# Two tiles of each layer's first bucket that load before the last scatters, four slot buffers, scatters without a bounds check, and a front without its surplus group

## The reference

```python
w = softmax(weight)                                   # 8 heads x 7 taps
x1[s, h] = sum over k of w[h, k] * x[s + k - 6, h]    # causal convolution, 24 numbers a head

do = x1 @ w_skip > 0                                  # first mixture layer, only these tokens
e  = argmax(x1 @ gate1);  g = softmax(...)[e]
x2 = x1 + do * g * (relu(x1 @ w1[e]) @ w2[e])         # 8 experts, 192 -> 1024 -> 192

e  = argmax(x2 @ gate2);  g = softmax(...)[e]         # second mixture layer, every token
out = g * sigmoid(x2 @ out_gate2)[e] * (relu(x2 @ w1'[e]) @ w2'[e])
```

## Time and profile before

| | us |
|---|---|
| median of 3 runs (lowest, highest) | 1117.85 (1116.25, 1118.25) |
| the profiled execution | 1117.96 |
| its span, first to last instruction | 1116.2 |
| PE busy in the span | 1048.8 |
| POOL busy in the span | 381.1 |
| mean granted PE clock | 0.976 of full |

### The profile page before, as it was taken

One profiled execution on the slowest core, in us unless ns is written; L12 is line 12 of the kernel. 1 busy time (PEld: TensorE's weight loads), 2 busy tenths in 40 slices (PEclk: granted clock), 3 DMA queues, 4 the chain that ended last, 5 costly groups with the idle time before them and its releaser, 6 DMA issues.

```text
span 1116.2 us, 32024 instructions
## 1 busy us (share of the span) xinstructions
PE 1048.8 (94%) x8478; PEld 988.4 (89%) x8479; DVE 704.9 (63%) x2258; ACT 528.4 (47%) x1190; POOL 381.1 (34%) x420
## 2 busy tenths in 40 slices
PE   7887747999999999999699999999999999999997
PEld 6666636999999999999599999999999999999997
DVE  1556654887878888888655555565656555565554
ACT  3445532444545454544245454554545455455443
POOL 2677773232323333333222232222323223223212
PEclk9999977999999999999899999999999999999999
DMA  7855334443433344344253343433434343323222
GB/s 209 241 184 156 101 121 117 98 101 71 96 75 93 89 97 98 82 95 110 71 131 81 75 114 65 113 81 79 113 79 111 64 101 93 65 58 73 61 60 49
DMA packets 252866, 110.90 MB, mean 99 GB/s; under 512 B 170515, under 2 KB 247814, under 8 KB 252848
## 3 DMA queue, kind: packets, MB, share of 16 engines
q1 hardware_dynamic: 210344, 62.19, 26.7%
q0 software_dynamic: 14560, 27.96, 7.1%
q10 hardware_dynamic: 27944, 20.57, 6.8%
HBM read 79.48 MB, written 33.08 MB: 101 GB/s over the span
## 4 chain that ended last, share of the span: by engine, by line
PE 83%; issue 7%; POOL 5%; DVE 2%; ACT 1%; DMA 1%; ACTq 1%; POOLq 0%; SPq 0%; DVEq 0%
PE bank L1104 32%; PE bank L1119 26%; PE bank L1126 12%; PE bank L1095 5%; POOL buckets L440 5%; PE bank L1066 2%; PE bank L1065 1%; PE bank L1054 1%; PE bank L1055 1%; PE bank L963 1%; PE bank L982 1%; DMA buckets<-rows,slot_i 0%; PE bank L1026 0%; ACT rows L527 0%; PE bank L1027 0%
## 5 line engine op out<-in xcount | busy, mean ns | idle before, releaser
L1119 PE MATMUL bank<-w,hh 128*128 128x384 f32 x1488 | 444.4, 361 | 0.4 <-DVE hl L821 0.4
L1126 PE MATMUL bank<-w,hl 128*128 128x192 f32 x1488 | 363.9, 255 | 0.0
L821 DVE SCALAR_TENSOR_TENSOR hl<-bank,hh 128x512 fp32r<-128x512 f32 x372 | 252.8, 690 | 126.7 <-ACT hh L615 123.9
L615 ACT ACTIVATE hh<-bank 128x512 fp32r<-128x512 f32 x372 | 221.6, 599 | 161.0 <-PE bank L1104 147.4
L1126 PEld LDWEIGHTS bank<-w,hl 128*128 128x128 f32 x1488 | 282.9, 191 | 0.0
L1119 PEld LDWEIGHTS bank<-w,hh 128*128 128x128 f32 x1488 | 280.4, 188 | 1.5 <-DVE hl L821 0.6
L466 POOL DMA_INDIRECT out<-y_rows,out_i x120 | 117.3, 978 | 413.4 <-DVE out_i L899 382.1
L1104 PE MATMUL bank<-xAh,w1h 128*128 128x256 f32 x744 | 222.5, 299 | 0.0
L1104 PE MATMUL bank<-xAh,w1l 128*128 128x256 f32 x744 | 210.2, 283 | 0.0
L1104 PE MATMUL bank<-xB,w1h 128*128 128x256 f32 x744 | 208.8, 281 | 0.0
L1104 PE MATMUL bank<-xAl,w1h 128*128 128x256 f32 x744 | 208.4, 280 | 0.0
(11 more groups left out here) (157 smaller groups left out, 1367.2 us busy)
## 6 DMA issues: line engine op xcount, KB each, us to landing
xblocks<-buckets SPq DMA_DIRECT2D x570, 32.0 KB, 1.8
xkeep<-buckets ACTq DMA_DIRECT2D x93, 196.0 KB, 2.7
xwin<-x SPq DMA_DIRECT2D x17, 672.0 KB
raw<-w_all SPq DMA_DIRECT2D x56, 192.0 KB
raw<-w_all SPq DMA_DIRECT2D x56, 128.0 KB
raw<-w_all SPq DMA_DIRECT2D x112, 64.0 KB
out<-y_rows,out_i POOLq DMA_INDIRECT x120
buckets<-rows,slot_i POOLq DMA_INDIRECT x112
```

Of the source, the lines that this page charges most:

```text
L615: nc.scalar.activation(hh[:, 2 * c:2 * c + 2, :].rearrange("p c t -> p (c t)"), bank[c][:], ACT.Relu).then_inc(s["h_high"], 1)
L821: nc.vector.scalar_tensor_tensor(hl[:, 2 * c:2 * c + 2, :].rearrange("p c t -> p (c t)"), bank[c][:], 0.0, h, ALU.max, ALU.subtract).then_ ...
L1119: return nc.tensor.matmul(bank[Y[h]][:, 0:2 * D], hh[:, j, t], w2[:, par, j, :, :].rearrange("p a d -> p (a d)"), start=(j == 0), stop=(j ...
L1126: last = nc.tensor.matmul(bank[Y[h]][:, 0:D], hl[:, j, t], w2[:, par, j, 0, :], start=False, stop=False)
```

## The change

- **Two tiles of the first bucket of each layer load early.** EARLY = 2. At the start POOL writes filler rows into the first 512 rows of buckets 0 and 8 (four DMAs of 128 x 392 floats) and waits for them. The bucket's fill level is raised to at least 512 rows: for bucket 0 after batch 2, for bucket 8 in `tables`. Tile 0 is then loaded without a condition, and `all_there` is asked for only from tile 2 on. `count_i` and the branch on `there` are gone.
- **Four slot buffers.** `slot_i` has GPB buffers, and DVE's wait ahead of L763 is gone. The first layer has a buffer of its own, `slot2_i`, and its wait is gone too.
- **Unchecked scatters.** The front's 112 scatters have no bounds check any more. The scatters of the layers keep theirs.
- **No surplus group.** The convolution, `rows_out` and windows of group 16 are gone, and so is the first layer's `send` in turn 0 (with its semaphores `copied` and `sent` raised in advance).
- **Ones matmuls.** 112 of them ahead of the first convolution, not 88, and 24 more between it and the first transposes.

```diff
-    CAP = N + T
+    EARLY = 2
+    CAP = N + (EARLY + 1) * T
-    MAXT = N // T + E
+    MAXT = N // T + E + EARLY
-        slot_i = sb("slot_i", [128, 2, WPG], I32)
+        slot_i = sb("slot_i", [128, GPB, WPG], I32)
+        slot2_i = sb("slot2_i", [128, SUB], I32)
...
-            sp.wait_ge(conv_ready, (B - 1) * GPB + 1)
-            load_windows(0, 0)
...
                 if m == 0:
-                    sp.wait_ge(counted, B - 1)
+                    sp.wait_ge(raised, 1)
+                    sp.wait_ge(prefilled, 16 * 2 * EARLY)
...
-                there = sp.value_load(count_i[0:1, m:m + 1], min_val=0, max_val=CAP)
-                with sp.If(there > T - 1):
-                    load_prep(0, m * E * CAP)
+                load_prep(0, m * E * CAP)
...
-                with sp.If(there < T):
-                    all_there()
-                    load_prep(0, m * E * CAP)
...
+                            with sp.If(g > EARLY - 1):
+                                all_there()
                             with sp.If(g > 0):
-                                all_there()
                                 sp.wait_ge(s["x_trans"], g)
                                 load_prep(g, off)
...
-                pool.dma_start(spare[:, n, :], weight_rev).then_inc(semaphore, 16)
+                pool.dma_start(spare[:, n, :], weight_rev).then_inc(semaphore, (48, 16)[n])
...
+            pool.wait_ge(consts_pool, 12)
+            for m in range(2):
+                for t in range(EARLY):
+                    pool.dma_start(bass.AP(buckets.tensor, (m * E * CAP + t * T) * ROW, [[SUB * ROW, 128], [1, SUB * ROW]]),
+                                   filler[:].rearrange("p s c -> p (s c)")).then_inc(prefilled, 16)
+            prime(pool, mix_sems[0]["copied"])
+            pool.wait_ge(prefilled, 16 * 2 * EARLY)
...
-                            out=buckets, out_offset=bass.IndirectOffsetOnAxis(ap=slot_i[0:W, q % 2, t:t + 1], axis=0),
-                            in_=rows[0:W, q, t, :], in_offset=None,
-                            bounds_check=NB * CAP - 1, oob_is_err=False).then_inc(scattered[q], 16)
+                            out=buckets, out_offset=bass.IndirectOffsetOnAxis(ap=slot_i[0:W, q, t:t + 1], axis=0),
+                            in_=rows[0:W, q, t, :], in_offset=None).then_inc(scattered[q], 16)
...
                             if m == 0:
-                                send(g, pieces.one)
+                                with pool.If(g > 0):
+                                    send(g, pieces.one)
...
-                    rows_out(n + 1, (q + 1) % GPB)
+                    if q < GPB - 1:
+                        rows_out(n + 1, q + 1)
+                    else:
+                        with act.If(b < B - 1):
+                            rows_out(n + 1, 0)
...
-                    dve.wait_ge(scattered[(q + 2) % GPB], b * (16 * WPG) + 16 * WPG * (1 if q < 3 else 2))
-                    nc.vector.tensor_copy(slot_i[0:W, q % 2, :], slot[0:W]).then_inc(slots_ready, 1)
+                    nc.vector.tensor_copy(slot_i[0:W, q, :], slot[0:W]).then_inc(slots_ready, 1)
...
-                with dve.If(b < B - 1):
-                    nc.vector.tensor_copy(count_i[:, 0:1], next_row[0:1, 0:1]).then_inc(counted, 1)
+                with dve.If(b > B - 3):
+                    with dve.If(b < B - 1):
+                        nc.vector.tensor_scalar(next_row[:, 0:1], next_row[:, 0:1], float(EARLY * T), None,
+                                                ALU.max).then_inc(raised, 1)
+                        dve.wait_ge(raised, 1)
...
-            with pe.Fori(0, 11):
-                for _ in range(8):
+            def warm(n):
+                for _ in range(n):
                     nc.tensor.matmul(bank[7][:, 0:128], ones[:], ones[:], start=True, stop=True)
+
+            with pe.Fori(0, 14):
+                warm(8)
             pe.wait_ge(win_zero, 3)
             for part in range(2):
                 conv(0, 0, part)
+            warm(24)
...
-                        conv(n + 1, (q + 1) % GPB, half)
+                        next_group(q, b, lambda n, q: conv(n, q, half))
```

More of the change, by code:

```diff
@@ L121, in program @@
         bucket_int = sb("bucket_int", [128, NB], I32)
-        count_i = sb("count_i", [1, 2], I32)
         tile_f = sb("tile_f", [1, 6, E])
@@ L154, in program @@
         hot, hot2 = hot_pad[:, WPG:2 * WPG, :], hot2_pad[:, SUB:2 * SUB, :]
-        consts_in, consts_pool, kern_in, kern_step, kern_out, halo_in, kern_e = map(sem, (
-            "consts_in", "consts_pool", "kern_in", "kern_step", "kern_out", "halo_in", "kern_e"))
+        consts_in, consts_pool, prefilled, kern_in, kern_step, kern_out, halo_in, kern_e = map(sem, (
+            "consts_in", "consts_pool", "prefilled", "kern_in", "kern_step", "kern_out", "halo_in", "kern_e"))
         toep_in = [sem("toep_in0"), sem("toep_in1")]
@@ L167, in program @@
             "scoreT_ready", "scoreT_copied", "scores_ready", "z_ready", "e_ready", "hot_ready", "rank_ready"))
-        slots_ready, route_step, ones_ready, counted, table_step, tables_ready, first_filled, filled = map(sem, (
-            "slots_ready", "route_step", "ones_ready", "counted", "table_step", "tables_ready",
+        slots_ready, route_step, ones_ready, raised, table_step, tables_ready, first_filled, filled = map(sem, (
+            "slots_ready", "route_step", "ones_ready", "raised", "table_step", "tables_ready",
             "first_filled", "filled"))
@@ L461, in send @@
                             nc.gpsimd.indirect_dma_start(
-                                out=buckets, out_offset=bass.IndirectOffsetOnAxis(ap=slot_i[:, 0, h:h + 1], axis=0),
+                                out=buckets, out_offset=bass.IndirectOffsetOnAxis(ap=slot2_i[:, h:h + 1], axis=0),
                                 in_=s_rows[:, h, :], in_offset=None,
@@ L775, in tables @@
                 if m == 0:
-                    nc.vector.tensor_tensor(count_i[:, 1:2], next_row[0:1, E:E + 1], bucket_row[0:1, E:E + 1],
-                                            ALU.subtract)
+                    nc.vector.tensor_scalar(next_row[:, E:E + 1], next_row[:, E:E + 1], float(E * CAP + EARLY * T),
+                                            None, ALU.max).then_inc(raised, 1)
                 step = Steps(table_step, 6 * m)
@@ L803, in _ @@
                 dve.wait_ge(tables_ready, m + 1)
+                dve.wait_ge(raised, 2)
                 def x_turn(n):
@@ L876, in places @@
                     step.after(a)
-                    dve.wait_ge(s["sent"], r * 32 + 16)
-                    nc.vector.tensor_tensor(slot_i[:, 0, 0:SUB], sl, flag[:, 0, :], ALU.add).then_inc(s["slots"], 1)
+                    nc.vector.tensor_tensor(slot2_i[:], sl, flag[:, 0, :], ALU.add).then_inc(s["slots"], 1)
                 def result(g):
@@ L1008, in scores_of, with next_group @@
                 last.then_inc(scores_ready, 1)
+            def next_group(q, b, part):
+                if q < GPB - 1:
+                    part(b * GPB + (q + 1), q + 1)
+                else:
+                    with pe.If(b < B - 1):
+                        part(b * GPB + (q + 1), 0)
             def last_group(q, b, part):
@@ L1042, in _ @@
             ranks_of(GPB * B - 1)
-            pe.wait_ge(rows_ready, GPB * B + 1)
             LG2 = bank[7][:, T:T + SUB * 2 * E].rearrange("p (t c) -> p t c", c=2 * E)
```

## The result

The changed kernel takes 1110.0 us, the median of 5 runs (1107.64 to 1111.2), against 1118.08 (1116.25 to 1118.25) for the kernel before on the same chip: ratio 0.9929, 95% interval 0.9915 to 0.9944. That is 8 us gained. The forecast was 1106.5 with 1097.0 to 1109.5 as its range, so the sign was right, the gain too large by 3.5 us, and the median lies just above the range. The profiled execution took 1109.96 us, its span 1108.2.

The account below looks back on a forecast made before the run. POOL's scatters pace the front, then tile 1's load waits for the last scatter; PE bounds the tiles after. Tile 2 moving from 198.91 to 187.4 gains 11.5, all else nothing: 1117.96 - 11.5 = 1106.5 us, range 1097 to 1109.5.

Parts of the forecast that it names:

- The surplus `send`: First layer, turn 0: removing two scatters and a copy on POOL gains nothing, as POOL is not the limit there.
- the second tile's early load and the tail of the front: Front to tile 2 of the first layer: tile 2 starts at 187.4 instead of 198.91, gain 11.5 us.
- at the higher I take 1.4: First layer, L1072 to tile 1: 1.4 us at PE's higher clock, instead of 2.52 at the lower.
- one plain period of 11.10: First layer: tile 1 takes 11.10 us, from its start at 176.3 to tile 2 at 187.4.
- Rival 2: Early load comes, but start 1.3 late (2.1 more) and clock lost in stall (1.1 more): 1107.5 to 1110, chance 0.10.
- tile 1's load: SP's queue behind the front: issued at 168.4, landed 4.36 us later at 172.8, leaving about 2.8 us of PE's stall.
- the unchecked scatter: POOL's scatter stream in the front: dropping the bounds check leaves the step unchanged at 1.29 us.
- Rival 1: Unchecked scatter is faster: 0.84 us per 0.01 off the step, up to 8.3 at 1.19; 1106.5 to 1098.2, chance 0.33.
- The front's 3.4 us: Tail of the front: tables and tile 0 earlier by 2.3 (no surplus group) plus 1.1 us (four slot buffers).
- The start: Start of POOL's scatters: 0.8 us earlier, between 1.3 earlier (ones matmuls hold clock) and 1.3 later (prefill traffic).
- Nothing in the change touches that work, so its time stands: PE's tiles from 198.9 to 543 us, busy throughout, one per 11.10 us: time unchanged.
- Is tile 2 in time?: Tile 2's load, after all scatters: landed at 181.1, wanted at 183.4; no delay, slack 2.3 us.

Follow-up runs that it names:

- e8: Changed kernel with tile 1 waiting for all scatters again, the rest of the change kept: 1116.37 us, ratio 0.9976.
- e7: Changed kernel with 76 ones matmuls on PE in the first layer's tile 0, ahead of the stalling rank matmuls: 1110.29 us, ratio 0.9922.
- e9: Changed kernel with an even expert's remaining weight pieces issued on SP behind the next expert's first tile load: 1108.11 us, ratio 0.9913.
- e10: e9 with tile 1's load also issued ahead of the bucket fills, as in e5: 1106.15 us, ratio 0.988.
- r1_checked: Changed kernel with the bounds check back on the front's 112 scatters: 1112.47 us, ratio 0.9938.
- e13: Changed kernel with the surplus group 16 back in the front: 1112.06 us, ratio 0.9943.
- r1_slots2: Changed kernel with two slot buffers and DVE's wait ahead of the slots again: 1112.38 us, ratio 0.9942.
- r1_again: The changed kernel run once more with no edit: 1109.76 us, ratio 0.9917 to the kernel before.
- e5: Changed kernel with SP's load of tile 1 issued right behind the tables, ahead of the filler DMAs: 1111.59 us, ratio 0.993.
- e12: e10 with the first layer's bucket fills 1 to 5 and six of the second layer's issued by POOL: 1103.98 us, ratio 0.986.
- r1_nowarm: Changed kernel without the additional ones matmuls (88 ahead of the first convolution, none behind): 1110.86 us, ratio 0.9929.
- e14: Kernel before with the early loads alone; surplus group, two slot buffers, checked scatters and 88 ones matmuls kept: 1117.73 us, ratio 0.9996.

## Why the prediction was right or wrong

**Right: the mechanism.** The last scatter was what held tile 1, and it no longer does; a shorter stall is left behind SP's own issue, as said. e8 shows the early load at some 6 us. In the profile tile 2 moves by 5.9 us, counted from the first scatter. The surplus `send`, the raised levels and the second layer's early tile cost nothing that shows: bucket 0 has the same tiles, and the second layer takes 532.82 us as before.

**Wrong: two terms of "the second tile's early load and the tail of the front"**, "at the higher I take 1.4" and "one plain period of 11.10". They took the clock as full behind the remaining stall. After 3.79 us of idle PE ran at 1.2 GHz (granted clock 0.50 from 174 to 178 us): 2.52 us to tile 1, 12.44 for it, 2.5 us in all. Rival 2 priced that at 1.1 us and counted it as unlikely; the earlier trace rows had it in plain sight, 12.35 us for the period behind the stall of before. e7, with the clock held, gives back 1.43 and 11.10. The forecast's own stall of 2.8 us would most likely not have saved the clock either: 2.70 us in e9 cost it.

**How the 3.5 us add up.** In the profile tile 0 comes 1.8 us earlier than forecast, tile 0 to L1092 takes 0.6 more, and the clock costs 2.5: tile 2 is 1.3 us late. Another 2.2 us are lost behind it. The clock is the largest term, and a better front than forecast hid more than half of it. It is not the whole cause: e7 holds the clock and its median is 1110.29, because tile 3 waits for SP's queue (below). e10 takes the stall and that wait away, and 1106.15 is close to the forecast. The range was also narrower than its terms: 1106.5 with 2.1 for a late start and 1.1 for the clock is 1109.7, above its end of 1109.5.

**Mis-sized: tile 1's load.** It was issued at 166.62 (168.4 expected), with tile 0 at 158.41 (160.2), but took 4.96 us to land, not 4.36, and PE reached L1092 11.5 us behind tile 0 and not 11.84; so the stall was 3.79 and not 2.8.

**Wrong, and in the kernel's favour: the unchecked scatter.** I took the step unchanged. Rival 1 was right: 0.96 against 0.98 us a scatter. r1_checked puts 2.5 us of tile 0 on it, of which 1.3 to 1.8 are the step and the rest mostly two single long scatters. My reason, that a scatter whose rows all lie out of bounds costs as much as one whose rows are all written, only shows that the outcome of the bounds test costs nothing, not that the test does. The step stays far above 1.19, where rival 1 would have ended. The branch price of the Trainium skill ("GPSIMD Engine Reference", 3.1 Elementwise), about 12 cycles an element, does not describe it: what goes is 0.02 us for 128 rows.

**The front's 3.4 us.** They became 4.7, counted from the first scatter, and the two profiles show them in three parts. ACT's copy of group 15 comes 1.7 us earlier (108.1 us behind the first scatter, 109.8 before): the step of the scatters. DVE's choice of group 15 comes 3.6 us earlier, so 1.9 more for the surplus group, where the forecast had 2.3. The slots come 4.7 earlier, so 1.1 more for the four buffers, as forecast. What exceeds 3.4 is therefore the step. Put back one by one, the parts cost 2.5 (r1_checked), 1.8 (e13) and 2.3 (r1_slots2), 6.7 in all. They are not terms of a sum: DVE's wait for the slots, for one, is 2.27 us where the choice comes early and 1.12 where it came late.

**The start.** The first scatter came at 29.91, 0.5 earlier than expected, which is partly luck: the same kernel had it at 30.68 in r1_again. The Trainium skill ("Trainium Kernel Development and Optimization", Key Constraints) has the queues of SP, ACT and POOL share the same 16 DMA engines. The trace fits it, but not where I looked: the tap matrix is only 0.28 us late; it is the second group's windows that come late (last section).

**Not foreseen: 2.3 us given back** between tile 2 and the second layer. "Nothing in the change touches that work, so its time stands" holds for the second layer. The first layer's stretch from tile 2 to 32 was 333.0 to 334.7 us in the profiles with no other cause, the passage 35.5 to 38.4, and the one profile of before is near the low end of both. Part of the gap is therefore the luck of one execution. Single periods of 11.2 to 11.7 us (0.51 us of issue ahead of L1115 at 355.92, for one) come and go from profile to profile: four in the changed kernel, two when it ran again, one of 11.22 us before. Their cause is open. No run was made on it.

**Left out: tile 3's load.** "Is tile 2 in time?" was asked of tile 2 alone. With tile 2 at 187.4 the sum needs tile 3 at 198.5; in the changed kernel its load is issued at 190.85 and it starts at 199.78, in e7 at 192.31 and 200.58. Tile 3 was the next wall: the changed kernel meets it by tenths of a us, so any further gain ahead of it would have been lost, as e5 and e7 show.

## What to carry to other kernels

When a stall gets shorter but does not go, the low clock behind it stays: take the period behind the stall from the trace before and keep it in the sum. When a load is moved up, follow the queue that issues it to the next loads, not only to the next tile: here eight weight DMAs ahead of tile 3's load swallowed 5.1 us, and their order gave it back. And try parts out of the full version as well as alone: the early load was worth 6 us in the new front and nothing that could be measured in the old one, though its profile has tile 1 4.5 us closer to tile 0 there.

## What the runs showed of the hardware that was not expected

**Late windows and the clock.** With the prefills, the second group's convolution waits for its halo windows in 13 of 15 profiles, up to 1.40 us. The DMA share from 9 to 11 us, where the prefills move, is 1.04 in the changed kernel and 0.55 before. In the one profile of before PE comes to that convolution at 17.01 and doesn't wait. That the prefills are the cause is inferred from this: no run takes them alone out. The convolution's start and the first scatter go together: 16.68 and 29.91 in the changed kernel, 17.15 and 30.39 in e10, 17.44 and 30.68 in r1_again, 17.89 and 31.20 in r1_checked, always 13.2 to 13.3 us apart. In e12, with a wait of 1.37 us, and without the extra ones matmuls already at one of some 0.5 us (r1_nowarm, e14; PE had idled 1.95 and 1.74 us just ahead of the transposes), the clock falls behind the wait and the distance is 14.9 to 15.1 us. e12's convolution and its window behind it:

```profile
17.98 2.19 PE L983 MATMUL bank<-xwin,toep 128*128 128x168 f32 x8 [1.37 <-DMA xhalo<-x]
```

```profile
17.00:19.00 2.00, 1.02 (x5) 1.02 (x6) 0.25 (x2) 0.71 (x2) 0.00 (x0) 0.86 0.87 217
19.00:21.00 2.00, 2.00 (x10) 1.88 (x9) 0.00 (x0) 0.00 (x0) 0.00 (x0) 0.50 1.14 348
```

So the late windows cost 0 to 1.4 us in waiting, and some 1.7 more where the clock goes with it. With the extra ones matmuls the clock held in 12 of 13 profiles, without them in neither of two.

**Single scatters of 1.4 to 1.5 us** occur in otherwise even streams, none to four in a profile, with nothing in the trace to name their cause.
